# Units 48 to 71 of a two-layer gated network as couples of 64-row tiles in two banks that swap

## The reference

```python
# layer 1
gate = 1.0 / (1.0 + np.exp(-(x @ w_gate)))
x = (gate * (x @ w_val)) @ w_out
# layer 2
y = ((x @ w_a) * (x @ w_b)) @ w_out2
```

## Time and profile before

| | us |
|---|---|
| median of 3 runs | 463.96 |
| lowest, highest | 463.11, 467.02 |
| the profiled execution | 463.46 |
| its span (first to last instruction) | 461.7 |
| TensorE busy | 456.5 (99%), 2527 matmuls |
| TensorE weight loads busy | 397.2 (86%) |
| VectorE, ScalarE, GpSimd busy | 206.0, 201.2, 88.1 |

### The profile page before, as it was taken

One profiled execution on the slowest core, in us unless ns is written; L12 is line 12 of the kernel. 1 busy time (PEld: TensorE's weight loads), 2 busy tenths in 40 slices (PEclk: granted clock), 3 DMA queues, 4 the chain that ended last, 5 costly groups with the idle time before them and its releaser, 6 DMA issues.

```text
span 461.7 us, 6673 instructions
## 1 busy us (share of the span) xinstructions
PE 456.5 (99%) x2527; PEld 397.2 (86%) x2527; DVE 206.0 (45%) x365; ACT 201.2 (44%) x370; POOL 88.1 (19%) x99
## 2 busy tenths in 40 slices
PE   8999999999999999999999999999999999999997
PEld 6888889898989989888889889989888888888886
DVE  8877786776465654343142253223232222322223
ACT  5965948658283745245253353213132222222222
POOL 4583232422403020102454260000000000000000
DMA  4979696452533460001322300000010000100001
GB/s 147 272 238 270 183 282 189 136 169 76 150 109 98 133 217 4 1 1 32 114 97 83 111 1 1 1 0 0 1 57 1 1 1 0 58 0 1 0 2 57
DMA packets 22005, 38.06 MB, mean 82 GB/s; under 512 B 2910, under 2 KB 16225, under 8 KB 21973
## 3 DMA queue, kind: packets, MB, share of 16 engines
q1 hardware_dynamic: 21605, 36.58, 26.1%
q10 hardware_dynamic: 208, 0.71, 0.5%
q0 software_dynamic: 160, 0.35, 0.3%
HBM read 35.55 MB, written 2.04 MB: 81 GB/s over the span
## 4 chain that ended last, share of the span: by engine, by line
PE 94%; ACT 2%; DMA 1%; DVE 1%; issue 1%; POOL 0%; DVEq 0%; POOLq 0%
PE bank L590 38%; PE bank L640 27%; PE bank L606 17%; PE bank L510 4%; PE bank L623 2%; PE bank L476 1%; PE bank L501 1%; ACT pt L742 1%; PE bank L524 1%; PE bank L566 1%; PE bank L485 1%; PE bank L536 1%; DMA f_row<-f_in 1%; DMA arow<-a_lo 0%; PE bank L448 0%
## 5 line engine op out<-in xcount | busy, mean ns | idle before, releaser
L1021 DVE TENSOR_TENSOR h_ff<-bank,s_ff 128x512 f32<-128x512 f32 x72 | 49.8, 691 | 131.5 <-PE bank L590 64.0
L806 ACT CAST h_hi<-h_ff 128x512 fp32r<-128x512 f32 x72 | 44.7, 620 | 135.7 <-PE bank L640 69.2
L1027 DVE TENSOR_TENSOR h_lo<-h_ff,h_hi 128x512 fp32r<-128x512 f32 x72 | 51.6, 717 | 96.1 <-ACT h_hi L806 96.1
L799 ACT ACTIVATE s_ff<-bank 128x512 f32<-128x512 f32 x72 | 43.1, 599 | 104.7 <-PE bank L623 54.0
L590 PE MATMUL bank<-xt,w_hi 128*128 128x512 f32 x240 | 79.0, 394 | 0.0
L590 PE MATMUL bank<-xt,w_lo 128*128 128x512 f32 x144 | 56.3, 391 | 0.0
L590 PEld LDWEIGHTS bank<-xt,w_hi 128*128 128x128 f32 x240 | 43.8, 188 | 8.6 <-DVE t_st L989 0.4
L640 PE MATMUL bank<-w_hi,h_hi 128*128 128x320 f32 x144 | 45.0, 312 | 0.0
L640 PE MATMUL bank<-w_lo,h_hi 128*128 128x320 f32 x144 | 44.4, 309 | 0.0
L640 PE MATMUL bank<-w_hi,h_lo 128*128 128x320 f32 x144 | 44.4, 309 | 0.0
L590 PE MATMUL bank<-xt,w_hi_end 128*128 128x512 f32 x120 | 39.3, 393 | 0.0
(11 more groups left out here) (153 smaller groups left out, 850.8 us busy)
## 6 DMA issues: line engine op xcount, KB each, us to landing
w_raw<-w_in SPq DMA_DIRECT2D x24, 544.0 KB, 3.9
vk<-vk_in SPq DMA_DIRECT2D x12, 344.0 KB, 3.6
levels<-a_scratch SPq DMA_DIRECT2D x7, 512.0 KB
k_both<-kq_in SPq DMA_DIRECT2D x21, 120.0 KB
q_blk<-kq_in SPq DMA_DIRECT2D x21, 120.0 KB
y<-rows_t SPq DMA_DIRECT2D x12, 160.0 KB, 1.9
q<-kq_in SPq DMA_DIRECT2D x10, 180.0 KB
osig_b<-o_in SPq DMA_DIRECT2D x8, 160.0 KB, 2.6
```

The source lines that it names most:

```text
L799: act.activation(s_ff[u % 2][:, :], up_bank(u, 0)[:, :], ACT.Sigmoid if u < UNITS // 2 else ACT.Copy).then_inc(act_s, 1)
L806: act.copy(h_hi[u % 2][:, :], h_ff[u % 2][:, :]).then_inc(act_h, 1)
L1021: dve.tensor_tensor(h_ff[u % 2][:, :], up_bank(u, 1)[:, :], s_ff[u % 2][:, :], ALU.mult).then_inc(dve_h, 1)
L1027: dve.tensor_tensor(h_lo[u % 2][:, :], h_ff[u % 2][:, :], h_hi[u % 2][:, :].bitcast(F32), ALU.subtract).then_inc(dve_hlo, 1)
```

## The change

All up products of units 48 to 71, and the down products of units 47 to 70, are made of 64-row matmuls in couples: one in rows 0 to 63 and one in rows 64 to 127 of the array, each into a bank of its own.

In `up_pair` (which takes two units at once, at the even one) a unit has a first and a second half. In the first, gate's upper rows (eight passes) are coupled with val's lower rows (eight passes); in the second, val's upper rows with gate's lower rows (seven each). Both row tiles add into the same two banks, and between the halves they swap them; the new semaphore pe_up_half says that a first half is complete. The order in a pair is first half of a, first half of a+1, second half of a, second half of a+1. Before each first half the stream waits for act_s and dve_h of the unit two before.

In `down_tiles` a down product is four groups of three couples: banks (1, 0), (3, 2), then with the row tiles swapped (0, 1), (2, 3). A group waits for the one two before it (pe_ob_first, pe_ob_half, pe_ob_last, pe_d). Down products come one unit later than before: after an odd unit u those of u-3 and u-2 (after unit 49 only 47's), and after unit 71 those of 68, 69 and 70 as tiles and 71's whole.

```diff
--- before.py
+++ after.py
@@ -188,6 +188,8 @@
...
         ld_q_own, pool_wup = sem("ld_q_own"), sem("pool_wup")
+        pe_up_half, pe_ob_first, pe_ob_half, pe_ob_last = (
+            sem(n) for n in ("pe_up_half", "pe_ob_first", "pe_ob_half", "pe_ob_last"))
...
@@ -592,38 +594,72 @@
                                    start=(j == 0), stop=(j == len(PASSES) - 1))
                 mm.then_inc((pe_g, pe_v)[gv], 1)
 
-            def up_whole(u, gv, first):
-
-                m, g, f = u // (NG * NF), u // NF % NG, u % NF
-                if first:
-                    if gv == 0 and f == 0:
-                        pe.wait_ge(dve_tr, BLK * (g + 1))
-                    if gv == 0 and g == 0:
-                        pe.wait_ge(*split_done(NF * m + f))
-                    free = u if u == PAIRED else u - 1
-                    pe.wait_ge((act_s, dve_h)[gv], free)
-                for j, (low, kt, xb) in enumerate(WHOLE):
-                    mm = pe.matmul(up_bank(u, gv)[:, :], w_part(low, f, (gv * 3 + kt) * P, P),
-                                   xt[:, xb * TOK + g * TG:xb * TOK + (g + 1) * TG],
-                                   start=(first and j == 0), stop=(not first and j == len(WHOLE) - 1))
-                if not first:
-                    mm.then_inc((pe_g, pe_v)[gv], 1)
-
-            def up_halves(u, first):
+            def up_part(u, gv, row, passes, first):
 
                 g, f = u // NF % NG, u % NF
-                for gv in range(2):
+                part = slice(row * KREM, (row + 1) * KREM)
+                for j, (low, kt, xb) in enumerate(passes):
+                    at = xb * TOK + g * TG
+                    side = x_twin[part, (g - 1) * TG:g * TG] if row and low and kt == 2 else xt[part, at:at + TG]
+                    mm = pe.matmul(up_bank(u, gv)[:, :], w_part(low, f, (gv * 3 + kt) * P, P)[part, :], side,
+                                   start=(first and j == 0), stop=(not first and j == len(passes) - 1))
+                    yield mm
+
+            def up_pair(a):
+
+                m, g, f = a // (NG * NF), a // NF % NG, a % NF
+                if f == 0:
+                    pe.wait_ge(dve_tr, BLK * (g + 1))
+                if a == PAIRED:
+                    pe.wait_ge(dve_tr, NCH)
+                    pe.wait_ge(act_s, a)
+                    pe.wait_ge(dve_h, a)
+                for first in (True, False):
+                    for u in (a, a + 1):
+                        if first and a > PAIRED:
+                            pe.wait_ge(act_s, u - 1)
+                            pe.wait_ge(dve_h, u - 1)
+                        low, high = (0, 1) if first else (1, 0)
+                        wait(pe, pe_up_half, 0 if first else u - PAIRED + 1)
+                        top = up_part(u, low, 0, PASSES if low == 0 else WHOLE, first)
+                        end = up_part(u, high, 1, WHOLE if high == 0 else PASSES, first)
+                        for mm0, mm1 in zip(top, end):
+                            pass
+                        if first:
+                            mm1.then_inc(pe_up_half, 1)
+                        else:
+                            mm0.then_inc(pe_v, 1)
+                            mm1.then_inc(pe_g, 1)
+
+            def down_tiles(u):
+
+                group, f = u // NF, u % NF
+                r = u % 2
+                pe.wait_ge(dve_hlo, u + 1)
+                if f == 0 and group:
+                    for tb in range(BLK):
+                        pe.wait_ge((act_row, dve_row)[tb % 2], 2 * group - 1 + tb // 2)
+                done = u - PAIRED + 1
+                for first, tbs in ((True, (1, 0)), (True, (3, 2)), (False, (0, 1)), (False, (2, 3))):
                     if first:
-                        pe.wait_ge((act_s, dve_h)[gv], u - 1)
-                        wait(pe, dve_tr, NCH if u == PAIRED + 1 and gv == 0 else 0)
-                for gv in range(2):
-                    part = slice(gv * KREM, (gv + 1) * KREM)
-                    side = (xt[part, 4 * TOK + g * TG:4 * TOK + (g + 1) * TG],
-                            x_twin[part, (g - 1) * TG:g * TG])[gv]
-                    mm = pe.matmul(up_bank(u, gv)[:, :], w_part(1, f, (gv * 3 + 2) * P, P)[part, :], side,
-                                   start=first, stop=not first)
-                    if not first:
-                        mm.then_inc((pe_g, pe_v)[gv], 1)
+                        last = u - PAIRED - (u - PAIRED) // NF
+                        wait(pe, (pe_ob_last, pe_d)[tbs[0] // 2], (last, u)[tbs[0] // 2] if done else 0)
+                    else:
+                        pe.wait_ge((pe_ob_first, pe_ob_half)[tbs[0] // 2], done + 1)
+                    for j, (h, low) in enumerate(((h_hi, 0), (h_hi, 1), (h_lo, 0))):
+                        for row, tb in enumerate(tbs):
+                            part = slice(row * KREM, (row + 1) * KREM)
+                            mm = pe.matmul(OB[tb][:, 0:DM], h[r][part, tb * P:(tb + 1) * P],
+                                           w_part(low, f, W1C, DM)[part, :],
+                                           start=(f == 0 and first and j == 0),
+                                           stop=(f == NF - 1 and not first and j == 2))
+                            if f == NF - 1 and not first and j == 2 and tb < BLK - 1:
+                                mm.then_inc(pe_ob, 1)
+                    if first:
+                        mm.then_inc((pe_ob_first, pe_ob_half)[tbs[0] // 2], 1)
+                    elif tbs[0] == 0 and f < NF - 1:
+                        mm.then_inc(pe_ob_last, 1)
+                mm.then_inc(pe_d, 1)
 
             def down(u):
 
@@ -694,13 +730,7 @@
                     up(u, 0)
                     up(u, 1)
                 elif u % 2 == 0:
-                    up_whole(u, 0, True)
-                    up_whole(u, 1, True)
-                    up_halves(u, False)
-                else:
-                    up_halves(u, True)
-                    up_whole(u, 0, False)
-                    up_whole(u, 1, False)
+                    up_pair(u)
                 if k == 2:
                     turn(n)
                     if n >= NCH - BLK:
@@ -711,8 +741,12 @@
                     if u:
                         down(u - 1)
                 elif u == UNITS - 1:
-                    for v in range(u - 2, u + 1):
-                        down(v)
+                    for v in range(u - 3, u):
+                        down_tiles(v)
+                    down(u)
+                elif u > PAIRED:
+                    for v in range(max(u - 3, PAIRED - 1), u - 1) if u % 2 else ():
+                        down_tiles(v)
                 elif u >= PAIRED - 1:
                     for v in range(u - 2, u) if u % 2 else ():
                         down(v)
```

## The result

| | before | the change |
|---|---|---|
| median us | 463.75 (4 runs) | 459.46 (4 runs) |
| lowest, highest | 463.11, 467.02 | 459.22, 459.62 |
| profiled execution, span | 463.46, 461.7 | 459.44, 457.7 |
| matmuls | 2527 | 3151 |
| first matmul of unit 45's down product to the last matmul | 134.66 | 130.54 |

A forecast was written before the change was run, and what follows sets the result against it. The prediction took the tensor engine's own stream as the bound: -4.6 for mode changes, +0.65 for couples, two stalls of 0.27, 0.1 at the end, -3.2 us after allowance, from 463.46 to 460.3 us; range 459.1 to 466.0.

The forecast's parts named there:

- The price of a visit: Units 48 to 71: each pair's change of tiling mode, in and out, costs 0.42 us; net -4.6 us.
- The price of a couple: Surplus of a couple over a whole matmul: 0 to 3 ns, taken as 1 ns, 0.65 us for 648 couples.
- Its own range: The forecast's range with the bounds on a couple's price: 459.2 to 461.9 us.
- Own waits: Down products' 94 waiting groups: awaited load may start at 0.65 us, needed at 0.77; 0.12 us slack, no cost.
- Other waits: Waits on other engines: 0.27 us each before units 51 and 63, 0.1 us before the last down product.
- The tenth for the cover of three couples: Down products: waits covered by only three couples may cost a tenth now and then, making the sum -3.2 us.
- issue: Rival: four instructions per couple meet a supply limit of 53 ns each, +13, so 473 us; chance 0.12.
- slow release: Rival: TensorE's own waits release beyond the 0.12 us slack, each 0.05 us costing 4.7: 465.0; chance 0.11.
- serial loads: Rival: a couple's two loads run one after the other in 288 down couples, +21, 481 us; chance 0.03.
- loads that wait for their own row tile: Rival: each of 648 couples takes load plus columns, +71, 531 us; chance 0.02.
- The pause belongs to the swap: Rival: the pause comes from swapping banks behind a wait and stays, +5 on before, 468.5 us; chance 0.04.
- faster by over 1%: Outcome below 459.3 us, holding the better case and the forecast's lower edge; chance 0.11.

The follow-up runs named there:

- whole down products: The changed kernel with every down product whole again, up products still in couples: 463.53 us, ratio 1.000 to before.
- a second visit: The kernel with whole down products, but in ten odd units' down products banks 0 and 1 made as tiles, banks 2 and 3 whole: 467.73 us.
- the kernel of whole passes: The kernel before with units 48 to 71 made of eight whole passes per product, no couples of halves: 463.65 us, ratio 1.003.
- the run with later down products: The kernel before with only the down products moved, after an odd unit those of u-3 and u-2: 464.68 us, ratio 1.002.
- the last product in tiles: The changed kernel with later row copies, and unit 71's down product in tiles as well: 459.86 us, ratio 0.992 to before.
- later row copies: The changed kernel with row copies of the groups ending at units 47 and 59 moved behind the next unit's s_ff and h_ff: 458.99, again 458.97 us.
- the run with unit 68's down product earlier: On top of later row copies, unit 68's down product moved ahead of the second halves of units 70 and 71: 458.81 us.
- the one with two queues: The kernel with later row copies and the last product in tiles, ScalarE issuing its two last-group row stores instead of SyncE: 459.75 us.

## Why the prediction was right and wrong

- **What bounded the kernel.** Right. The visits to 64-row mode were the only idle time in the rewritten part, and removing them is the whole gain: whole down products bring them back and the time of before with them, a second visit adds as much again.
- **The price of a visit.** 0.42 us read from one pair; 0.40 and 0.42 in the two runs that add visits. Right within 0.02. In the stream of before it was 0.44: the pair of 10.79 against 10.81 for the kernel of whole passes less its two further steps of 0.2267.
- **The price of a couple.** Here the sum failed. The prediction put it "between nothing and the 3 ns that a step of 0.23 and a rounded 0.2285 leave open" and took 1 ns, 0.65 us in all. It measured nothing. In the change the couples of units 52 and 53 start at 347.35 (the third) and 353.47 (the thirtieth), 27 steps of 0.2267 us, and whole passes in before have the same step, (341.15 - 339.79) / 6:

```profile
339.79 0.62 PE L606 MATMUL bank<-xt,w_hi 128*128 128x512 f32 x2
...
341.15 0.39 PE L606 MATMUL bank<-xt,w_hi 128*128 128x512 f32 x1
```

The prediction's 0.2285 was no clean step: it is the mean of 13, of which the first five, behind the change from 320 to 512 columns, take 0.229 to 0.236, and so do the six behind a visit. Taken for all 30 steps it made a pair without a visit 10.37 us, where the kernels whose couples stay together have 10.35, and the visit 0.02 us too cheap. The pair was forecast at 10.42, 1 ns a couple included, and is 10.34: 1.0 us over twelve pairs, all of the miss of 0.9 and a little more. Of that 0.65 is the price of the couple, 0.2 the visits, and 0.1 the pairs whose couples stand some 50 ns apart: they are 0.013 us shorter than 10.353.
- **Its own range.** With 0 to 3 ns for a couple the sum gives 459.6 to 461.5 and not 459.2 to 461.9, so by its own bounds the prediction shut out what was measured.
- **A charge per tile.** The second tile of a couple starts 3 to 69 ns behind the first and the step is no longer for it. The 4 ns per further tile of the Trainium skill ("TensorE: Matmul & The Clock Gate", Part 3, Measured speedup vs the span model), which would have made 462.3, do not hold in a stream of couples.
- **Own waits.** Right: 0.05 us to release, nothing to see in the change, 0.33 us each when uncovered.
- **Other waits.** Right in place and cause, 0.31 us each where 0.27 was forecast. Entering the mode cost 0.21 us, as forecast. At the end the last down product starts 0.35 us later than 36 down couples would have it, and its first step is 0.25 us instead of 0.15: 0.45 in all, where the forecast had 0.31. The forecast made it of a change of mode (0.21) and a remainder of waiting; by the run with later down products, which has 0.44 us there without any change of mode, all of it is the wait for h_lo of unit 71, and with the last product in tiles, where no change of mode is left, the rewritten part stays at 130.01 us.
- **The tenth for the cover of three couples** was not needed.

The sum with measured terms: 12 x (10.34 - 10.79) = -5.4; entry +0.21; two pauses +0.62; the end +0.45; the last five pairs at 10.35 in place of 10.34 +0.06: -4.1, and the rewritten part is 4.11 us shorter.

The rivals: issue, slow release, serial loads and loads that wait for their own row tile are each excluded by a run or by the step of 0.147 us for four instructions. "The pause belongs to the swap" is excluded by the 24 swaps of the ups and the 94 waiting groups of the downs without one.

The chances were set too narrow. 0.11 for "faster by over 1%" was too little for a forecast 1.4 us under that line with an error bar on one side only. The working also set 460.3, reckoned from the profiled execution of before, against a line of 459.3 reckoned from its median, which is 0.5 us higher.

## What to carry to other kernels

Count changes of tiling mode before tiles: a change costs 0.20 to 0.22 us here, about as much as one whole matmul of 512 columns (0.227), so a trick that saves two steps and needs a visit of its own gains nothing, and pays only when the whole stretch stays in one mode. When two row tiles must swap banks, the second half can start at the earliest 0.47 us after the start of the first half's last matmul (0.31 to complete it, 0.05 to release the wait, 0.11 for the load), and other work should fill that; three couples of 320 columns were enough. And in a last product let the banks finish one by one, since the stores behind them need their time from the first one on.

## What the hardware showed that I had not expected

- How far apart the two matmuls of a couple start is not fixed by the kernel: up to 69 and 61 ns in two executions of the change, up to 42 with later row copies, never over 4 in the run with unit 68's down product earlier and in the one with two queues. The step of the couples is 0.2267 us in all of them, once settled. What sets the distance is not shown.
- Behind a change of mode, and behind a change from 320 to 512 columns, five or six steps are 2 to 9 ns longer before the step settles at 0.2267, for whole passes as for couples. Where the two of a couple stand some 50 ns apart, only about two steps are.
- TensorE took instructions at one each 30 ns for 7 us without falling behind.
- Four stores of 160 KB took 3.65 to 3.72 us from the first issue to the end in all kernels, on one queue or on two. Their packets fill 2.0 to 2.1 us of it.
